# Weight splits of the first group moved to earlier steps, clock fillers taken out of the first three tiles

## The chip, the cores and the metric

One program on one core of a Trainium2 chip, launched once. The metric is device time in microseconds from start to end of the program. The engines are TensorE (PE), VectorE (DVE), ScalarE (ACT), GpSimd (POOL) and SyncE (SP), which only issues DMAs here. Each runs its own instructions in order and waits on semaphores for the others.

## The reference

Three layers, one behind the other, all float32:

```
# 1. attention with a decaying state, 4 batches, 8 heads, 768 positions, 48 wide
for t in range(S):
    cur = einsum('bhd,bhe->bhde', u[None] * kt, vt)
    y[:, :, t] = einsum('bhd,bhde->bhe', rt, state + cur)
    state = w[None, :, :, None] * state + einsum('bhd,bhe->bhde', kt, vt)
# 2. gated layer, 3072 tokens x 384, 1536 hidden
gate = 1 / (1 + exp(-(x @ w_gate)))
x = (gate * (x @ w_val)) @ w_out
# 3. eight experts, each token to the one with the largest logit
logits = normalized(x) @ normalized(expert_emb).T / tau
out[mask] = gate_w[mask] * (relu(x[mask] @ w1[e]) @ w2[e])
```

## The kernel before

**Tiles and groups.** The 3072 tokens are 24 tiles of 128 (6 per batch). Three tiles make a group; there are 8 groups, 0 to 7. The gated layer works on a group at a time, in 12 steps (`hidden_step`, f = 0 to 11, 128 hidden columns each), and then projects the three tiles (`project`, 12 chunks each). Between the steps of a group the attention of the next group's tiles is worked in: `att_of` gives step f the stage (f - 1) mod 4 of one of three tiles. Stage 0 scales k and r (`scale_k`, `scale_r` on VectorE; the k_tok product L575 and the two bonus products on GpSimd), stage 1 is the scores on TensorE (L1255, L1262) and the masks and the state on VectorE (L935 to L954), stage 2 is the output (L1278, L1286), the bonus (L588 on GpSimd) and the sum of both (L963, L969 on VectorE), stage 3 turns it (L1292) and splits it (L737 on ScalarE, L973 on VectorE). Group 0 has no earlier group: its tiles T=0, 1, 2 are worked alone before step 0 (the opening). Beside group 0's steps run tiles T=3, 4, 5.

**Split matmuls.** Every matmul of layer 2 is made of three, with each float32 operand split into a high part, as the matmul's fp32r type rounds it, and the remainder. A step has 18 of them (L1332): per three chunks of 128 rows, for gate and value, high x high, high x low and low x high. A step's chain is: TensorE, the sigmoid (L745, ScalarE), the product with the value (L1081, VectorE, called the gate below), the high part of the hidden row (L749, ScalarE) and its low part (L618, GpSimd). TensorE's step f waits for the gate of step f - 2, since they share PSUM banks; the sigmoid of step f waits for L618 of step f - 2.

**Weights of layer 2.** They come as pieces: g0 to g5 (w_gate), v0 to v5 (w_val), each 256 hidden columns wide and so first used by step f = 2j, o0 to o5 (w_out, two chunks of the projection each), and t0 to t5 (w_out turned, from which 12 small column products on TensorE, `logit_columns`, L1302, work out the router's weights). A piece is loaded by SP into a room ("s0", "h", "l3", ...; `PIECES` has the order and the room), which must be free of its former tenant. ScalarE copies its high part (`make_hi`, L796), then VectorE (g, v: `make_lo`, L1124) or GpSimd (o: L600) subtracts it for the low part; both together are called the split below. Three tables say at which step of group 0 the queue of each engine has which piece, behind the step's own work: `HI_AT` (ScalarE), `LO_AT` (VectorE), `LO_O_AT` (GpSimd). The step's own work on VectorE and GpSimd includes the attention stage; on GpSimd attention comes before L618, on VectorE it comes behind the gate. Step f = 2j on TensorE waits for the later of g_j's and v_j's VectorE splits (`lo_count`).

**The opening's order.** On VectorE, ahead of tile 0's stage 1, stand the squares of the expert embeddings, their scaling (L989 to L992) and the copy of the turned embeddings (L994). Then for each tile: scale_k of the next, the split of g0 or v0, stage 2, scale_r of the next, stage 3, stage 1 of the next. Stage 1 ends with the sum L957, which waits for GpSimd's bonus products. On TensorE: stage 1, two logit columns, stage 2, two more, stage 3 and four filler matmuls on the identity (`keep_clock`, L1375), which write a bank nobody reads.

## Time and profile before

| | us |
|---|---|
| three runs | 877.86, 878.61, 879.29 |
| median | 878.61 |
| the profiled execution | 877.35 |
| its span | 875.6 |
| mean granted TensorE clock | 0.975 |
| TensorE busy | 837.6 (96%) |
| VectorE busy | 440.1 (50%) |
| GpSimd busy | 423.1 (48%) |
| ScalarE busy | 297.2 (34%) |

The span is what the profile covers; the execution's own time has what lies around it, 1.75 us. In the chain of work that ended last TensorE has 88% of the span. The span in 40 slices of 21.9 us, in tenths busy:

```profile
PE   6778899999999999999999999998999999999995
DVE  6566545545545545545545543377367267265100
PEclk8688899999999999999999999999999999999998
DMA  9643212212212212212212210136344354354110
```

TensorE falls short of 9 tenths in the first five slices (0 to 109 us) and at the turn to the experts. The granted clock is under 9 tenths in the same first slices.

### The profile page before, as it was taken

To read this page: it belongs to the slowest core of one execution; us is meant where nothing else is said; L and a number is where in the kernel's file an instruction comes from. 1 tells how busy PE (TensorE), PEld (TensorE's weight loads), DVE (VectorE), ACT (ScalarE), POOL (GpSimd) and SP (SyncE) were. 2 spreads that over 40 slices of the span, in tenths; PEclk is the share of its full clock that TensorE was granted. 3 is DMA by queue.
4 is the path that set the end of the run, shared out by engine and by line. 5 is a ranking of instruction groups with operands and counts; after the bars stand their busy time and mean duration, and the time that the engine had idled before them with its cause. 6 is when DMAs were issued, how large, how long until landed. Compare 5 with 4: busy or idle time off the path is not lost.

```text
span 875.6 us, 20375 instructions
## 1 busy us (share of the span) xinstructions
PE 837.6 (96%) x7466; PEld 792.2 (90%) x7467; DVE 440.1 (50%) x1051; ACT 297.2 (34%) x610; POOL 423.1 (48%) x452
## 2 busy tenths in 40 slices
PE   6778899999999999999999999998999999999995
PEld 6777899999999999999999999987999989989995
DVE  6566545545545545545545543377367267265100
ACT  1143223223223223223223214333544444454442
POOL 3465516516516516516516513336566466466544
PEclk8688899999999999999999999999999999999998
DMA  9643212212212212212212210136344354354110
GB/s 279 218 149 112 74 48 82 69 48 79 71 48 76 75 48 75 75 49 74 76 48 75 69 47 19 38 117 197 109 144 142 109 156 143 98 157 141 50 36 30
DMA packets 78421, 82.04 MB, mean 94 GB/s; under 512 B 5816, under 2 KB 75648, under 8 KB 78352
## 3 DMA queue, kind: packets, MB, share of 16 engines
q1 hardware_dynamic: 65200, 60.29, 23.1%
q10 hardware_dynamic: 9216, 9.55, 3.8%
q0 software_dynamic: 3936, 11.23, 3.4%
q8 instruction: 49, 0.80, 0.4%
q14 instruction: 20, 0.16, 0.1%
HBM read 69.83 MB, written 12.01 MB: 93 GB/s over the span
## 4 chain that ended last, share of the span: by engine, by line
PE 88%; DVE 4%; issue 2%; ACTq 2%; POOL 2%; ACT 1%; DMA 1%; POOLq 0%; DVEq 0%
PE ps L1332 33%; PE ps L1353 16%; PE ps L1435 13%; PE ps L1420 13%; PE ps L1443 3%; PE ps L1255 2%; PE ps L1278 1%; DVE weights L1124 1%; PE ps L1262 1%; PE ps L1292 1%; PE ps L1400 1%; PE ps L1286 1%; PE ps L1375 1%; ACTq L370 1%; POOL weights L600 1%
## 5 line engine op out<-in xcount | busy, mean ns | idle before, releaser
L1332 PE MATMUL ps<-x_groups,weights 128*128 128x384 f32 x1728 | 321.9, 342 | 12.2 <-DVE weights L1124 12.2
L1332 PEld LDWEIGHTS ps<-x_groups,weights 128*128 128x128 f32 x1728 | 303.3, 191 | 14.9 <-issue 13.1
L618 POOL TENSOR_TENSOR hT<-gate,hT 128x384 fp32r<-128x384 f32 x96 | 104.1, 1087 | 144.4 <-ACT hT L749 144.4
L1353 PE MATMUL ps<-weights,hT 128*128 128x392 f32 x864 | 160.6, 344 | 0.0
L1353 PEld LDWEIGHTS ps<-weights,hT 128*128 128x128 f32 x864 | 152.6, 188 | 0.4
L1435 PE MATMUL ps<-weights,hT 128*128 x672 | 124.2, 339 | 1.7 <-ACT h_f L854 1.7
L1420 PE MATMUL ps<-weights,x_groups 128*128 (+1 forms) x504 | 122.8, 397 | 1.2 <-issue 1.2
L1081 DVE TENSOR_TENSOR gate<-ps,gate 128x384 f32<-128x384 f32 x96 | 53.5, 557 | 135.4 <-PE ps L1332 129.0
L1435 PEld LDWEIGHTS ps<-weights,hT 128*128 128x128 f32 x672 | 115.9, 188 | 2.0 <-issue 1.9
L1420 PEld LDWEIGHTS ps<-weights,x_groups 128*128 128x128 f32 x504 | 92.6, 188 | 20.5 <-issue 1.7
L1067 DVE CAST weights<-staged 128x768 fp32r<-128x768 f32 x56 | 49.3, 881 | 93.5 <-PE ps L1420 54.9
L749 ACT CAST hT<-gate 128x384 fp32r<-128x384 f32 x96 | 49.3, 514 | 124.1 <-DVE gate L1081 124.1
L1069 DVE TENSOR_TENSOR weights<-staged,weights 128x768 fp32r<-128x768 f32 x60 | 80.5, 1344 | 3.5 <-ACT weights L791 1.4
L623 POOL TENSOR_TENSOR top<-top,one_half 128x1 f32<-128x1 f32 x24 | 13.5, 563 | 134.9 <-ACT row L758 134.9
L745 ACT ACTIVATE gate<-ps 128x384 f32<-128x384 f32 x96 | 47.2, 491 | 90.5 <-PE ps L1332 77.4
L704 POOL TENSOR_TENSOR hT<-h_f,hT 128x512 fp32r<-128x512 f32 x56 | 72.2, 1308 | 2.7 <-ACT h_f L854 1.8
L758 ACT ACTIVATE row<-x 128x384 f32<-128x384 f32 x24 | 12.6, 527 | 117.3 <-DVE x L1001 117.3
L836 ACT ACTIVATE A_room<-ps 128x512 f32<-128x512 f32 x56 | 33.5, 599 | 46.4 <-PE ps L1420 45.5
L688 POOL COPY dest<-Z 128x1 int32 x28 | 9.4, 336 | 74.8 <-ACT k_in L859 74.8
L859 ACT COPY k_in<-ps 128x384 f32<-128x384 f32 x28 | 13.4, 478 | 92.0 <-PE ps L1435 92.0
L692 POOL DMA_INDIRECT out<-k_in,dest x28 | 29.9, 1066 | 23.7 <-POOL dest L688 22.2
L682 POOL TENSOR_TENSOR x_groups<-kT,x_groups 128x384 fp32r<-128x384 f32 x29 | 32.9, 1134 | 16.0 <-ACT kT L831 15.9
(183 smaller groups left out, 973.0 us busy)
## 6 DMA issues: line engine op xcount, KB each, us to landing
staged<-in_moe_w SPq DMA_DIRECT2D x60, 384.0 KB, 3.4
r_in<-routed ACTq DMA_DIRECT2D x30, 192.5 KB, 2.4
rk_raw<-in_rt SPq DMA_DIRECT2D x21, 256.0 KB, 3.6
rk_raw<-in_kt SPq DMA_DIRECT2D x21, 256.0 KB, 3.9
...
```

What stands on the lines that cost most here:

```text
L618: g.tensor_tensor(hT_lo[:, f, :], gate[:, f % 2, :], hT_hi[:, f, :].bitcast(F32), ALU.subtract).then_inc(hlo_ready, 1)
L704: g.tensor_tensor(eh_lo[:, c, :], h_f[:, c, :], eh_hi[:, c, :].bitcast(F32), ALU.subtract).then_inc(ehlo_ready, 1)
L745: s_.activation(gate[:, f % 2, :], ps[:, BG[f % 2], 0:GT], ACT.Sigmoid).then_inc(sig_ready, 1)
L749: s_.copy(hT_hi[:, f, :], gate[:, f % 2, :]).then_inc(hhi_ready, 1)
L836: s_.activation(h_rows[:, q * 512:(q + 1) * 512], ps[:, BH[q], :], ACT.Relu).then_inc(relu_ready, 1)
L1067: ve.tensor_copy(hi, raw).then_inc(ehi_step, 1)
L1069: ins = ve.tensor_tensor(lo, raw, hi.bitcast(F32), ALU.subtract)
L1081: ve.tensor_tensor(gate[:, f % 2, :], ps[:, BV[f % 2], 0:GT], gate[:, f % 2, :], ALU.mult).then_inc(h_ready, 1)
L1332: ins = te.matmul(ps[:, bank[f % 2], 0:GT], wt[:, c, fs], x[:, half, c, :], start=(c == 0 and m == 0), stop=(c == KC - 1 and m == 2))
L1353: ins = te.matmul(ps[:, BX2[i], 0:XW], h[:, f, ts], wt[:, f, :], start=(f == 0 and m == 0), stop=(f == FC - 1 and m == 2))
L1420: ins = te.matmul(ps[:, BH[q], :], x[:, c, :], columns(buf, o + c * EF + q * 512, 512), start=(c == 0 and m == 0), stop=(c == KC - 1 and m ...
L1435: ins = te.matmul(ps[:, BO, 0:DM], h[:, c, :], columns(buf, o + c * DM, DM), start=(ready is ehf_ready and c == 0 and m == 0), stop=(ready ...
```

## The change

Four things, no arithmetic among them:

1. The tables of group 0. The g and v splits stand at earlier steps than before on ScalarE and VectorE, the o splits at later steps than all but the last g and v ones. The o pieces now wait for the rooms s0, s1 and h instead of x0 to x2, and SP's order of loads follows.
2. The opening on VectorE. Stage 1 of tile 0 comes ahead of the scaling of the embeddings; the copy of the turned embeddings comes behind tile 0's stage 3; the splits of g0 and v0 stand ahead of the next tile's stage 1 instead of ahead of stage 2; the sum (`sum_bonus`) is taken out of stage 1 for these tiles, and for tiles 1 and 2 stands ahead of it. The embeddings lie in another buffer for that.
3. The opening on TensorE. The embeddings are turned behind tile 0's stage 3; the 12 logit columns come in tiles 1 and 2 (3, 2, then 3, 2, 2); the fillers of the three tiles are gone. The 16 + 8 fillers ahead of tile 0 stay.
4. ScalarE no longer waits for o2's split ahead of tile 3's stage 3, since no w_out piece lies in that room now.

```
-    HI_AT = {1: "g2 o0", 2: "o1 v2", 3: "o2 g3", 4: "v3", 5: "v4 o3", 6: "g4 o4", 7: "g5", 8: "v5 o5"}
-    LO_AT = {0: "g1 v1", 1: "g2", 3: "v2", 4: "g3 v3", 5: "v4", 7: "g4 g5", 8: "v5"}
-    LO_O_AT = {2: "o0 o1", 3: "o2", 6: "o3 o4", 8: "o5"}
+    HI_AT = {0: "g2 v2", 2: "g3", 3: "v3 v4", 4: "g4", 5: "o0 o1", 6: "g5 v5", 7: "o2 o3", 8: "o4", 9: "o5"}
+    LO_AT = {0: "g1 v1", 1: "g2 v2", 3: "g3", 4: "v3 v4", 5: "g4", 7: "g5 v5"}
+    LO_O_AT = {6: "o0 o1", 8: "o2 o3", 10: "o4", 11: "o5"}
...
-            load_pieces(PIECES[:17])
+            load_pieces(PIECES[:14])
             fetch(sp, 0, 3)
             fetch_v(sp, 0, 3)
-            load_pieces(PIECES[17:20])
+            load_pieces(PIECES[14:18])
             fetch(sp, 0, 4)
-            load_pieces(PIECES[20:21])
+            load_pieces(PIECES[18:19])
             fetch_v(sp, 0, 4)
-            load_pieces(PIECES[21:23])
+            load_pieces(PIECES[19:20])
             fetch(sp, 0, 5)
+            load_pieces(PIECES[20:23])
             fetch_v(sp, 0, 5)
             load_pieces(PIECES[23:])
...
                 if stage == 3:
-                    if isinstance(T, int) and T == TPG:
-                        act.wait_ge(*lo_count("o", 2))
                     act.wait_ge(y_turned, T + 1)
...
             hidden_step(0, 0)
+            for kind, j in pieces_at(HI_AT, 0):
+                make_hi(kind, j)
             batches(act, step)
...
-            attention(0, 0, 0, 1, 0)
             for i in range(TPG):
+                if i:
+                    make_lo("gv"[i - 1], 0)
+                    sum_bonus(i)
+                attention(0, i, i, 1, 0)
+                if i == 0:
+                    sum_bonus(0)
                 if i + 1 < TPG:
                     scale_k(0, i + 1)
-                    make_lo("gv"[i], 0)
+                if i == 0:
+                    scale_embeddings()
                 attention(0, i, i, 2, 0)
                 if i + 1 < TPG:
                     scale_r(0, i + 1)
                 attention(0, i, i, 3, 0)
-                if i + 1 < TPG:
-                    attention(0, i + 1, i + 1, 1, 0)
+                if i == 0:
+                    dve.wait_ge(en_t, 1)
+                    ve.tensor_copy(enT[:, :, :], ps[:, BX, 0:KC * E].rearrange("p (c e) -> p c e", c=KC)).then_inc(enT_ready, 1)
...
+            chunk = 0
             for i in range(TPG):
-                attention(0, i, i, 1)
-                if i == 0:
-                    turn_embeddings()
-                    pe.wait_ge(enT_ready, 1)
-                for c in range(4 * i, 4 * i + 2):
-                    logit_columns(c)
-                attention(0, i, i, 2)
-                for c in range(4 * i + 2, 4 * i + 4):
-                    logit_columns(c)
-                attention(0, i, i, 3)
-                keep_clock(BX2[1], 4)
+                for stage, chunks in ((1, 3), (2, 2), (3, 2)):
+                    attention(0, i, i, stage)
+                    if i == 0 and stage == 3:
+                        turn_embeddings()
+                        pe.wait_ge(enT_ready, 1)
+                    if i > 0 and (stage < 3 or i == TPG - 1):
+                        for c in range(chunk, chunk + chunks):
+                            logit_columns(c)
+                        chunk += chunks
             hidden_step(0, 0, 0, first=True)
```

In the changed kernel VectorE's lines stand 6 lower (L1124 is L1130), GpSimd's 1, TensorE's 13.

How the order moves, at two places. First GpSimd from step 6 of group 0 to the start of step 9. `hT` is the low part L618, `weights` a w_out split, `bonus` the bonus product of T=4, `k_tok` the k product of T=5. Before:

```order
L618 TENSOR_TENSOR hT<-gate,hT 128x384 x2
L600 TENSOR_TENSOR weights<-staged,weights 128x2x384 x2
L588 TENSOR_TENSOR bonus<-v_in,bonus_sum 128x384
L618 TENSOR_TENSOR hT<-gate,hT 128x384 x2
L600 TENSOR_TENSOR weights<-h_f,weights 128x2x384
L575 TENSOR_TENSOR k_tok<-k_in,pow_tok 128x8x48
```

Changed:

```order
L619 TENSOR_TENSOR hT<-gate,hT 128x384 x2
L601 TENSOR_TENSOR weights<-staged,weights 128x2x384 x2
L589 TENSOR_TENSOR bonus<-v_in,bonus_sum 128x384
L619 TENSOR_TENSOR hT<-gate,hT 128x384 x2
L601 TENSOR_TENSOR weights<-h_f,weights 128x2x384
L601 TENSOR_TENSOR weights<-staged,weights 128x2x384
L576 TENSOR_TENSOR k_tok<-k_in,pow_tok 128x8x48
```

The two splits ahead of the bonus are o0 and o1 instead of o3 and o4; ahead of k_tok there are two splits (o2, o3) instead of one (o5).

Second, VectorE in steps 1 to 3 of group 0. `gate` is the gate of a step, `weights` a g or v split, `kT` and `rT` T=3's scaled k and r, `A_room` the state and the masks, `bonus` the sums of T=3's output. Before:

```order
L918 TENSOR_TENSOR kT<-rk_raw,pow_k 128x512
L924 TENSOR_TENSOR rT<-rk_raw,pow_r 128x512
L1124 TENSOR_TENSOR weights<-first_room,weights 128x3x256
L1081 TENSOR_TENSOR gate<-ps,gate 128x384
L946 TENSOR_TENSOR A_room<-ps,Z 128x192
...
L963 TENSOR_TENSOR bonus<-ps,bonus 128x2x4x48
L969 TENSOR_TENSOR bonus<-ps,bonus 64x4x48 x2
L1124 TENSOR_TENSOR weights<-first_room,weights 128x3x256
L1081 TENSOR_TENSOR gate<-ps,gate 128x384
```

Changed:

```order
L924 TENSOR_TENSOR kT<-rk_raw,pow_k 128x512
L930 TENSOR_TENSOR rT<-rk_raw,pow_r 128x512
L1130 TENSOR_TENSOR weights<-first_room,weights 128x3x256 x2
L1087 TENSOR_TENSOR gate<-ps,gate 128x384
L952 TENSOR_TENSOR A_room<-ps,Z 128x192
...
L969 TENSOR_TENSOR bonus<-ps,bonus 128x2x4x48
L975 TENSOR_TENSOR bonus<-ps,bonus 64x4x48 x2
L1130 TENSOR_TENSOR weights<-staged,weights 128x3x256
L1087 TENSOR_TENSOR gate<-ps,gate 128x384
```

v2's split, which stood behind the bonus sums of step 3, now stands beside g2's in step 1, and g3's (from `staged`) has its place in step 3.

## Rows read from the trace of the kernel before

**Rows 1.** Windows, group 0 and group 1; busy us of PE, PEld, DVE, ACT, POOL, clock, DMA share, GB/s

```profile
43.76:128.85 85.09, 72.67 (x708) 69.52 (x708) 46.49 (x94) 26.95 (x51) 41.88 (x33) 0.90 0.32 98
128.85:194.79 65.94, 65.94 (x709) 63.52 (x708) 34.73 (x106) 18.96 (x41) 30.01 (x30) 1.00 0.22 66
```

**Rows 2.** Timeline of PE, steps 4, 6, 8: start, us, [idle before <-releaser]

```profile
66.89 5.46 PE L1332 MATMUL ps<-x_groups,weights 128*128 128x384 f32 x18 [5.80 <-DVE weights L1124]
...
77.39 3.39 PE L1332 MATMUL ps<-x_groups,weights 128*128 128x384 f32 x18 [1.58 <-DVE weights L1124]
...
90.83 4.50 PE L1332 MATMUL ps<-x_groups,weights 128*128 128x384 f32 x13 [4.57 <-DVE weights L1124]
```

**Rows 3.** Chain that ended last: start, us; steps 4 and 8 of group 0, one of group 1

```profile
66.89 5.46 PE ps L1332 x18
...
90.83 5.44 PE ps L1332 x18
...
139.48 3.33 PE ps L1332 x18
```

**Rows 4.** Timeline of POOL and DVE ahead of step 4

```profile
58.70 3.73 POOL L600 TENSOR_TENSOR weights<-group_room,weights 128x768 fp32r<-128x768 f32 x2
...
63.32 0.56 DVE L963 TENSOR_TENSOR bonus<-ps,bonus 128x384 f32<-128x384 f32 x1 [2.64 <-POOL bonus L588]
...
64.58 2.17 DVE L1124 TENSOR_TENSOR weights<-first_room,weights 128x768 fp32r<-128x768 f32 x1
```

**Rows 5.** Timeline of group 0: prices of splits, masks' last write, step 3, L618

```profile
54.85 1.76 DVE L1124 TENSOR_TENSOR weights<-first_room,weights 128x768 fp32r<-128x768 f32 x1
...
56.61 3.40 PE L1332 MATMUL ps<-x_groups,weights 128*128 128x384 f32 x18
...
57.71 1.02 POOL L618 TENSOR_TENSOR hT<-gate,hT 128x384 fp32r<-128x384 f32 x1 [0.22 <-ACT hT L749]
...
58.20 0.75 DVE L954 TENSOR_TENSOR Z<-Z,w_pow 128x192 f32<-128x192 f32 x1
...
78.58 1.50 DVE L924 TENSOR_TENSOR rT<-rk_raw,pow_r 128x512 f32<-128x512 f32 x1
...
89.72 0.96 DVE L1124 TENSOR_TENSOR weights<-h_f,weights 128x768 fp32r<-128x768 f32 x1
```

**Rows 6.** DMA issues, 40 to 110 us: KB each, median us to landing

```profile
staged<-in_moe_w_out SPq DMA_DIRECT2D x2, 384.0 KB, 3.9
```

**Rows 7.** DMA issues, 0 to 30 us: KB each, median us to landing

```profile
h_f<-in_moe_w_gate SPq DMA_DIRECT2D x1, 384.0 KB, 14.6
```

**Rows 8.** Windows, fillers of tile 0 and end of the first stall; columns as in rows 1

```profile
22.00:24.00 2.00, 1.23 (x6) 1.23 (x7) 1.59 (x4) 0.29 (x1) 1.32 (x3) 0.50 1.09 350
...
66.00:68.00 2.00, 1.11 (x4) 1.14 (x5) 0.74 (x1) 0.00 (x0) 0.00 (x0) 0.50 0.03 10
```

**Rows 9.** Timeline of the opening: scores of tile 0, embeddings, first read, logit columns

```profile
14.56 0.63 PE L1262 MATMUL ps<-v_in,k_tok 64*64 64x48 f32 x32
...
14.73 0.14 DVE L989 TENSOR_SCALAR tiny<-tiny 8x1 f32<-8x1 f32 x1 [0.75 <-POOL tiny L579]
...
17.48 0.35 DVE L944 COPY A_room<-ps 128x192 f32<-128x192 f32 x1
...
20.24 1.46 PE L1302 MATMUL ps<-enT,first_room 128*64 128x8 f32 x24
```

**Rows 10.** Chain that ended last, the opening: transposes of tiles 0, 1, 2, fillers

```profile
22.77 0.90 PE ps L1292 x3
23.68 1.71 PE ps L1375 x8
...
32.62 0.90 PE ps L1292 x3
...
41.50 0.90 PE ps L1292 x3
```

More of the change, by code:

```diff
@@ L67, in fused_kernel @@
               ("t", 4, "x1"), ("t", 5, "x2"), ("g", 1, "h"), ("v", 1, "l3"), ("g", 2, "l4"), ("v", 2, "l5"),
[2 rows of a table removed]
[2 rows of a table added]
     ROOM_OF = {(kind, j): room for kind, j, room in PIECES}
-    HI_SEQ = [("g", 0), ("v", 0), ("g", 1), ("v", 1), ("g", 2), ("o", 0), ("o", 1), ("v", 2), ("o", 2), ("g", 3),
-              ("v", 3), ("v", 4), ("o", 3), ("g", 4), ("o", 4), ("g", 5), ("v", 5), ("o", 5)]
+    HI_SEQ = [("g", 0), ("v", 0), ("g", 1), ("v", 1), ("g", 2), ("v", 2), ("g", 3), ("v", 3), ("v", 4), ("g", 4),
+              ("o", 0), ("o", 1), ("g", 5), ("v", 5), ("o", 2), ("o", 3), ("o", 4), ("o", 5)]
     LO_SEQ = [("g", 0), ("v", 0), ("g", 1), ("v", 1), ("g", 2), ("v", 2), ("g", 3), ("v", 3), ("v", 4), ("g", 4),
               ("g", 5), ("v", 5)]
-    HI_AT = {1: "g2 o0", 2: "o1 v2", 3: "o2 g3", 4: "v3", 5: "v4 o3", 6: "g4 o4", 7: "g5", 8: "v5 o5"}
-    LO_AT = {0: "g1 v1", 1: "g2", 3: "v2", 4: "g3 v3", 5: "v4", 7: "g4 g5", 8: "v5"}
-    LO_O_AT = {2: "o0 o1", 3: "o2", 6: "o3 o4", 8: "o5"}
+    HI_AT = {0: "g2 v2", 2: "g3", 3: "v3 v4", 4: "g4", 5: "o0 o1", 6: "g5 v5", 7: "o2 o3", 8: "o4", 9: "o5"}
+    LO_AT = {0: "g1 v1", 1: "g2 v2", 3: "g3", 4: "v3 v4", 5: "g4", 7: "g5 v5"}
+    LO_O_AT = {6: "o0 o1", 8: "o2 o3", 10: "o4", 11: "o5"}
     PRE, SPLIT = len(HI_SEQ), len(LO_SEQ)
-    RING = 6
+    RING = 8
     assert PRE == NWO + 2 * NWG and SPLIT == 2 * NWG and EPC % 2 == 0
@@ L154, in fused_kernel @@
         y = bonus[:, :, :].rearrange("p h d -> p (h d)")
-        enc = A_room[0:E, 0:DM]
         bonus_sum = sb("bonus_sum", [P, H])
@@ L165, in fused_kernel @@
         row = sb("row", [P, 2, ROW])
+        enc = row[0:E, 1, 0:DM]
         prio = sb("prio", [P, E])
@@ L913, in _, with sum_bonus @@
             w128 = w_pow[:, 7, :]
+            def sum_bonus(T):
+                dve.wait_ge(rk_step, T * 2 + 2)
+                ve.tensor_reduce(bonus_sum[:, :], bonus[:, :, :], AX_X, ALU.add).then_inc(sum_ready, 1)
             def scale_k(b, c):
@@ L955, in attention @@
                                          ALU.mult).then_inc(z_ready, 1)
-                    dve.wait_ge(rk_step, T * 2 + 2)
-                    ve.tensor_reduce(bonus_sum[:, :], bonus[:, :, :], AX_X, ALU.add).then_inc(sum_ready, 1)
+                    if not isinstance(T, int) or T >= TPG:
+                        sum_bonus(T)
                 elif stage == 2:
@@ L987, in _, with scale_embeddings @@
             ve.tensor_reduce(tiny[0:E, 1:2], x2[0:E, 0:DM], AX_X, ALU.add).then_inc(en_squares, 1)
-            dve.wait_ge(en_norm, 1)
-            link(ve.tensor_scalar(tiny[0:E, 2:3], tiny[0:E, 5:6], 1e-6, None, ALU.add))
-            link(ve.tensor_tensor(tiny[0:E, 3:4], tiny[0:E, 2:3], tiny[0:E, 0:1], ALU.mult))
-            link(ve.reciprocal(tiny[0:E, 4:5], tiny[0:E, 3:4]))
-            ve.tensor_scalar(enc[:, :], enc[:, :], tiny[0:E, 4:5], None, ALU.mult).then_inc(en_ready, 1)
-            dve.wait_ge(en_t, 1)
-            ve.tensor_copy(enT[:, :, :], ps[:, BX, 0:KC * E].rearrange("p (c e) -> p c e", c=KC)).then_inc(enT_ready, 1)
+            def scale_embeddings():
+                dve.wait_ge(en_norm, 1)
+                link(ve.tensor_scalar(tiny[0:E, 2:3], tiny[0:E, 5:6], 1e-6, None, ALU.add))
+                link(ve.tensor_tensor(tiny[0:E, 3:4], tiny[0:E, 2:3], tiny[0:E, 0:1], ALU.mult))
+                link(ve.reciprocal(tiny[0:E, 4:5], tiny[0:E, 3:4]))
+                ve.tensor_scalar(enc[:, :], enc[:, :], tiny[0:E, 4:5], None, ALU.mult).then_inc(en_ready, 1)
             def choose(G, i):
@@ L1380, in _ @@
             keep_clock(BC, 8)
+            chunk = 0
             for i in range(TPG):
-                attention(0, i, i, 1)
-                if i == 0:
-                    turn_embeddings()
-                    pe.wait_ge(enT_ready, 1)
-                for c in range(4 * i, 4 * i + 2):
-                    logit_columns(c)
-                attention(0, i, i, 2)
-                for c in range(4 * i + 2, 4 * i + 4):
-                    logit_columns(c)
-                attention(0, i, i, 3)
-                keep_clock(BX2[1], 4)
+                for stage, chunks in ((1, 3), (2, 2), (3, 2)):
[7 more added lines that the diff above has]
+                        chunk += chunks
+            assert chunk == FC
             hidden_step(0, 0, 0, first=True)
```

4 rows, old and new, of the table PIECES are left out of this document.

## The prediction

> **What bounds the kernel now.** Two stretches lie before the point from which TensorE never waits: the opening (0 to 43.76 us, three attention tiles, one after the other) and group 0 (43.76 to 128.85). I read first the windows by group: group 0 takes 85.09 us, group 1, with the same matmuls, 65.94 us, with TensorE busy all of it at a granted clock of 1.00 [rows 1]. So at most 19.2 us can be won in group 0, and nothing behind it, since later groups are already full.
>
> Second, TensorE's timeline in group 0: it idles 5.80 us ahead of step 4, 1.58 ahead of step 6 and 4.57 ahead of step 8, always for a VectorE split (L1124) [rows 2], 11.95 us together. Third, the chain: the two long stalls leave the clock down, so step 4 takes 5.46 us and step 8 5.44, where a step costs 3.33 [rows 3]; the granted clock there is 0.50, that is 1.2 GHz, after the idle time of 60 to 66 us [rows 8]. That is 2.13 + 2.11 = 4.24 us more. A 1.58 us gap costs no clock: step 6 takes 3.39 [rows 2].
>
> Why step 4 starts late is seen on GpSimd and VectorE: two output splits (3.73 us) stand ahead of the bonus product L588, VectorE's L963 waits for it (2.64 us), and v2's split, queued behind L963, ends only at 66.75, when step 4 starts [rows 4]. The stall ahead of step 8 is the same with o3, o4 and g4.
>
> **Group 0, what goes.** In the changed order g2 and v2 are split in step 1, g3 in step 3, v3 and v4 in step 4, g4 in step 5, g5 and v5 in step 7, so none of the three steps finds its split behind a bonus wait of the same step. GpSimd has no output split before step 6. All three stalls and both slow steps go: 11.95 + 4.24 = **16.2 us**.
>
> **Group 0, what comes.** The splits still cost VectorE the same; 1.76 us each where GpSimd works beside them, 0.96 where it rests [rows 5]. They now stand ahead of other things:
> - Step 1: v2's split is added behind g2's. T=3's masks, whose last write ends at 58.95 now, end 1.76 later, at 60.7; TensorE is there at 60.01 [rows 5]. Wait 0.7 to 1.2, I take 0.9. GpSimd has lost its 3.73 us there, so the bonus of T=3 is then in time.
> - Step 4 to 5: gate, L973, two splits (3.5), gate, scale_k, scale_r (1.0 + 1.5, the second [rows 5]). From step 4's start: 3.3 + 0.6 + 0.8 + 3.5 + 0.6 + 2.5 = 11.3, against steps 4 to 6 and a turn of 0.3 on TensorE, 10.3 to 10.4. Wait 0.9 for T=4's scores. Step 6's own split ends at about 6.5, ahead of 7.0.
> - Steps 6 to 8: o0 and o1 stand ahead of T=4's bonus as o3 and o4 do now. From step 6: scale_r ends at 4.3, g4's split and the gate at 6.6, copy and L618 1.6 (L618 1.02 [rows 5]), splits 3.7, bonus 0.8, L963 and L969 1.25: 14.0 to 14.2, against TensorE at step 8's end 13.1. Its transposes wait 1.0, no longer its hidden steps.
> - Steps 8 to 9: a new place. Now one output split (o5) lies between L618 of step 8 and T=5's k_tok product, then two (o2, o3). From step 6's start as above: g5 and v5 0.96 each after 14.2, gate, copy, L618: 18.2; splits 3.7 to 4.8; k_tok 1.0: 22.9 to 24. TensorE wants k_tok at 21.7 (13.1, the wait of 1.0, the turn 0.3, steps 9 and 10, 0.6 of score matmuls). Wait 1.9 (1.2 to 3).
> - Small ones, steps 2 and 11: 0.3. The last output split ends about 1 us ahead of its use in the projection: nothing, or 1 if late.
>
> Sum of new waits 0.9 + 0.9 + 1.0 + 1.9 + 0.3 = **5.0 us** (3 to 8), none near the length that took the clock down. Group 0 gains 16.2 − 5.0 = 11.2.
>
> The w_out loads now form a chain, each waiting for a consumed room. A load of this kind lands in 3.9 us [rows 6]; at that the copies of o3 and o5 hold ScalarE for a few us, which delays sigmoids of steps 8 and 10 but no step two behind them. SP's other moves (T=3's loads up to 10 us earlier, since the three w_out loads ahead of them are gone; T=4's loads behind v5) stay inside slack.
>
> The split price needs a rule weighed. The row says 1.76 beside a GpSimd instruction and 0.96 alone [rows 5], a slowing of both, not a block. The Trainium skill (SBUF — State Buffer, Who interferes with whom) says that a VectorE instruction with two SBUF inputs and a GpSimd instruction that reads SBUF hold a shared port as an exclusive lock, so the later one fully blocks. By that a split behind a 1.0 us product would take about 1.96, the waits of steps 1 and 4 would grow by some 0.2 and 0.4, and the sum would be 0.6 us less gain.
>
> **The opening.** Tile 0: scores are there at 15.19, but VectorE, in the embedding work from 14.73 on, starts tile 0's first read at 17.48 [rows 9]. Now that read comes first: 2.29 earlier. The four embedding operations (2.2 us from 14.73 to 16.94) then stand ahead of L963 instead, and the 1.1 us split and enT's copy leave it: 15.2 + 1.9 (reads, masks, sum) + 0.6 (kT) + 2.2 = 19.9, plus 1.25 gives the transposes at 21.2, where they stand at 22.77 [rows 10]: 1.6 earlier (0.8 to 2.5).
>
> Tile to tile: now 9.85 and 8.88 us between transposes, 1.71 of each in fillers on the chain [rows 10]. Changed, VectorE sets it: L973 done 2.0 after the transposes start, split 1.0 to 1.6, sum 0.5, four mask and state operations 1.55: 5.1 to 5.7; TensorE's second stage 1.1; L963, L969 1.25: 8.1 for the second turn. In the first, TensorE also waits for enT's copy (at 2.2), and 36 logit matmuls at a rate of 24 in 1.46 us [rows 9] follow its scores (4.15 + 2.2 = 6.35), so second stage from 6.3: 8.7 to 9.6. I take 9.2 and 8.3: 0.65 and 0.6 earlier. The last fillers ahead of step 0: L973 is the limit anyhow, 0.3. Opening: 1.6 + 0.65 + 0.6 + 0.3 = **3.1 us** (1 to 5).
>
> **Sum.** 11.2 + 3.1 = 14.3 us. The profiled execution took 877.35 (span 875.6), so 863.05 for it; the median of the three runs is 878.61, 1.26 above, so **864.3**.
>
> **Rivals.**
> - *The clock.* The fillers ran at 0.50 with TensorE 1.23 of 2 us busy [rows 8]; they may still be what brings it to full speed for each tile's second stage. Without them the second stage costs about 1.0 more in each tile, and one of the new waits may grow past 3 us and take the clock down once (2.1 + 1.5). For it: four waits share GpSimd and VectorE. Against: no single one is worked out above 3. Gain 8 to 11, time 869. In a sentence of its own: the Trainium skill (TensorE: Matmul & The Clock Gate, What's actually happening) has the default state as throttled and activity as what releases it, by which removing fillers speaks against this change. Chance 0.17.
> - *The clock stays up from the last tile into step 0*, as logit matmuls fill what was idle, and port contention is milder: steps 0 and 1 save 1.8, the waits 1 to 2. Gain 17.5, time 861. Chance 0.10.
> - *The chain of w_out loads decides (slower).* ScalarE's queue is in order: behind the copy of o3 (step 7) and of o5 (step 9) stand the sigmoids that TensorE's banks wait for. In the opening a load of the same size took 14.6 us to land [rows 7]. At that, two places lose 14.6 − 3.9 = 10.7 each, less 2 of slack: +19.4 − 14.3 = +5, time 884. It turns slower from a landing of 3.9 + (14.3 + 2) / 2 = 12 us. Against it: by step 6 the loads are few, and landed in 3.9 [rows 6]. Chance 0.03.
> - *It moves nothing,* because another wait of equal length already stands behind each (the bonus product, TensorE's own transposes): the time stays at 878.6. Against: each wait named by the profile is for a split. Chance 0.02.
>
> **How the numbers follow.** Forecast 0.68, rivals as above. The likeliest gives 864.3; its own bounds (new waits 3 to 8, opening 1 to 5) give 860.5 to 869, which also takes in most of the two clock cases. 0.2% is 1.8 us, about what a measurement of this kernel can tell from no change. Faster 0.95, same 0.02, slower 0.03.
>
> **What would show it.** In the changed profile TensorE's idle time for splits in group 0 is under 1 us instead of 12; step 0 starts at about 40.7; group 0 lasts about 74; no 18-matmul step behind step 0 takes over 4 us; new idle times of 1 to 2 us appear ahead of L1255/L1262, L1278 and the transposes, the longest for T=5's k_tok. A stall of over 3 us with a 0.50 clock behind it, or ScalarE waiting long for a w_out load, would make the prediction wrong; so would an opening that is no shorter.

## The result and the profile after

| | before | changed |
|---|---|---|
| median of the runs made side by side, us | 878.95 (877.86 to 879.74, 4 runs) | 869.56 (869.07 to 871.41, 4 runs) |
| profiled execution, us | 877.35 | 869.66 |
| its span, us, mean granted clock | 875.6, 0.975 | 867.6, 0.977 |

The ratio is 0.9898, 95% interval 0.9879 to 0.9916: 9 us faster, where 14.3 were forecast. The median lies 0.56 us above the upper end of the stated range (860.5 to 869; the bounds given for its parts add up to 869.4), and within 0.6 us of the 869 of the rival "the clock".

The page of the changed kernel, its row for the hidden steps (columns: busy us, mean ns | idle time ahead, its releaser). Before, idle time for VectorE splits was 12 us [rows 2]:

```profile
L1345 PE MATMUL ps<-x_groups,weights 128*128 128x384 f32 x1728 | 320.2, 341 | 0.2 <-DVE weights L1130 0.2
```

Windows of group 0 and group 1 in the changed kernel, columns as in [rows 1]:

```profile
42.24:118.81 76.57, 71.80 (x710) 68.48 (x709) 47.04 (x94) 27.18 (x52) 41.64 (x33) 0.93 0.37 110
118.81:184.80 65.99, 65.99 (x709) 63.56 (x708) 34.77 (x107) 18.96 (x41) 30.02 (x30) 1.00 0.22 66
```

Group 0 went from 85.09 to 76.57 us (8.5 won, 11.2 forecast), and group 1 is as it was. It starts 10 us earlier than before, of which the profiled execution keeps 8 at its end. The rest, from group 1's start on, which no edit here touches, took 746.9 us in the profile of before, 748.8 in this one and 747.1 to 749.4 in those of the experiments: a profile of one execution is good to some 2 us there, and the profile of before has the lowest of all.

The timeline of TensorE in group 0 of the changed kernel: the waits that are left.

```profile
42.35 8.27 PE L1345 MATMUL ps<-x_groups,weights 128*128 128x384 f32 x36
50.88 3.39 PE L1345 MATMUL ps<-x_groups,weights 128*128 128x384 f32 x18 [0.25 <-DVE weights L1130]
...
59.34 0.26 PE L1291 MATMUL ps<-v_in,A_room 64*64 64x48 f32 x2 [0.67 <-issue]
...
71.58 0.69 PE L1268 MATMUL ps<-rT,kT 64*64 64x64 f32 x32 [1.08 <-DVE rT L930]
...
81.24 0.55 PE L1305 MATMUL ps<-ident,bonus 128*128 128x128 f32 x3 [0.76 <-DVE bonus L975]
...
89.92 0.69 PE L1268 MATMUL ps<-rT,kT 64*64 64x64 f32 x32 [1.86 <-DVE rT L930]
90.78 1.09 PE L1275 MATMUL ps<-v_in,k_tok 64*64 64x48 f32 x16 [0.16 <-POOL k_tok L576]
91.80 5.93 PE L1345 MATMUL ps<-x_groups,weights 128*128 128x384 f32 x18
```

None of the three long stalls of [rows 2] is left. In their place stand 0.25 + 0.67 + 1.08 + 0.76 + 1.86 + 0.16 = 4.8 us of short waits (the 0.25 ahead of step 2 is not new: 0.24 stood there before). For the 0.67 the profile names no releaser; VectorE's last write of T=3's masks ends at 59.24 us, just ahead of 59.34. But the last row, step 11, takes 5.93 us and not 3.4. The windows around it say why (the clock is the last number but two):

```profile
88.00:90.00 2.00, 0.14 (x5) 0.08 (x8) 1.86 (x1) 0.00 (x0) 2.00 (x2) 1.00 0.85 222
90.00:92.00 2.00, 1.84 (x49) 1.61 (x50) 0.27 (x1) 1.22 (x2) 1.92 (x3) 0.63 0.83 237
92.00:94.00 2.00, 2.00 (x7) 2.00 (x8) 1.67 (x5) 0.52 (x1) 2.00 (x3) 0.50 0.60 191
```

Behind the wait of 1.86 us the granted clock goes from 1.00 (2.4 GHz) to 0.50 (1.2 GHz), and step 11 runs at half speed for most of its time. What TensorE waited for there is on VectorE and GpSimd (timelines of both):

```profile
85.81 1.84 DVE L924 TENSOR_TENSOR kT<-rk_raw,pow_k 128x512 f32<-128x512 f32 x1
87.57 2.29 DVE L930 TENSOR_TENSOR rT<-rk_raw,pow_r 128x512 f32<-128x512 f32 x1
```

```profile
85.23 1.87 POOL L601 TENSOR_TENSOR weights<-h_f,weights 128x768 fp32r<-128x768 f32 x1
87.06 2.26 POOL L601 TENSOR_TENSOR weights<-staged,weights 128x768 fp32r<-128x768 f32 x1
89.28 1.45 POOL L576 TENSOR_TENSOR k_tok<-k_in,pow_tok 128x384 f32<-128x384 f32 x1
```

scale_k (L924) ends at 87.65, 0.55 us behind the first GpSimd split (87.10); scale_r (L930) ends at 89.86, 0.54 behind the second (89.32). In the opening, at 30.63 us with GpSimd at rest, the same L930 takes 0.69. So the two output splits o2 and o3 made scale_r late. They made k_tok (L576) late too: it stands behind both and ends at 90.73. The 0.16 that the timeline shows for it is only what was left of that wait. Steps 9 and 10 end at 88.06 us. Had scale_r been in time, the scores could have started then and the k_tok matmuls about 0.5 later, and TensorE would have waited 1.3 to 2.1 us for k_tok instead of 1.86 + 0.16 (an estimate from these rows; the 1.3 is with L601 and L576 as short as alone, 1.85 and 1.02 us).

The opening. Timeline of TensorE in the changed kernel, from tile 0's transposes on:

```profile
20.25 0.90 PE L1305 MATMUL ps<-ident,bonus 128*128 128x128 f32 x3 [2.46 <-DVE bonus L975]
23.44 1.13 PE L1268 MATMUL ps<-rT,kT 64*64 64x64 f32 x32 [1.88 <-DVE enT L1149]
25.32 2.09 PE L1315 MATMUL ps<-enT,first_room 128*64 128x8 f32 x36
27.35 1.11 PE L1291 MATMUL ps<-first_room,A_room 64*64 64x48 f32 x32
...
29.24 0.91 PE L1315 MATMUL ps<-enT,first_room 128*64 128x8 f32 x13
...
30.93 0.90 PE L1305 MATMUL ps<-ident,bonus 128*128 128x128 f32 x3
...
36.80 1.15 PE L1291 MATMUL ps<-first_room,A_room 64*64 64x48 f32 x32 [1.06 <-DVE A_room L941]
...
38.73 1.45 PE L1315 MATMUL ps<-enT,group_room 128*64 128x8 f32 x24
40.14 0.90 PE L1305 MATMUL ps<-ident,bonus 128*128 128x128 f32 x3
```

Against [rows 10], with tiles 1 and 2 from the changed kernel's chain: tile 0's transposes 22.77 → 20.25, tile 1's 32.62 → 31.0, tile 2's 41.50 → 40.2, step 0 43.76 → 42.35. What tile 0 won, 2.5 us, shrinks to 1.4. The chain says what tile 1's scores waited for:

```profile
19.38 1.28 ACT L802
...
20.87 1.46 ACT weights L795 x2
22.33 0.39 ACT x_groups L736
...
22.74 0.56 DVE x_groups L979
23.30 0.10 DVE enT L1149
```

VectorE's copy of enT stands behind L979, which waits for ScalarE's L736, which stands behind two high-part copies (L795) and a table load (L802). And the granted clock is 0.50 from 16 to 46 us. That shows in the second stages of tiles 1 and 2, from the first L1291 to the logit matmuls behind: 27.35 to 29.24 and 36.80 to 38.73, 1.9 us each. In the profile of before the same stage of tile 1 took 1.08 us:

```profile
28.97 0.68 PE L1278 MATMUL ps<-first_room,A_room 64*64 64x48 f32 x32 [0.93 <-DVE A_room L935]
...
30.05 1.12 PE L1302 MATMUL ps<-enT,group_room 128*64 128x8 f32 x24
```

The granted clock from 28 to 30 us is 1.00 in the profile of before and 0.50 in the changed kernel's.

ScalarE's waits between 60 and 110 us, for the rival about the w_out loads (us in total, times, longest):

```profile
ACT weights L795 <- DMA h_f<-in_moe_w_out: 4.0, 1, 4.0
ACT weights L795 <- DMA staged<-in_moe_w_out: 3.0, 1, 3.0
```

The loads do hold ScalarE, as worked out, but no hidden step waits for a sigmoid: no such wait stands in TensorE's timeline.

### The profile page after: what moved, and what is told of

Same layout as the page of the kernel before. It is cut to its first block, busy times and chain, and to the rows that moved or that the text cites. A ratio compares the mean times of both kernels' runs of the same rounds, so it can differ in the third digit from the quotient of the medians.

```text
span 867.6 us, 20325 instructions
## 1 busy us (share of the span) xinstructions
PE 835.4 (96%) x7442; PEld 789.1 (91%) x7443; DVE 440.1 (51%) x1051; ACT 297.4 (34%) x610; POOL 423.6 (49%) x452
## 4 chain that ended last, share of the span: by engine, by line
PE 86%; DVE 4%; POOL 3%; issue 2%; ACTq 2%; ACT 1%; DMA 1%; POOLq 0%; DVEq 0%; SPq 0%
PE ps L1345 32%; PE ps L1366 17%; PE ps L1448 14%; PE ps L1433 13%; PE ps L1456 3%; PE ps L1291 2%; PE ps L1268 1%; PE ps L1299 1%; PE ps L1275 1%; PE ps L1413 1%; ACTq L370 1%; PE ps L1305 1%; POOL weights L601 1%; PE ps L1315 1%; DVE weights L1130 1%
## 5 line engine op out<-in xcount | busy, mean ns | idle before, releaser
L1087 DVE TENSOR_TENSOR gate<-ps,gate 128x384 f32<-128x384 f32 x96 | 53.5, 557 | 129.2 <-PE ps L1345 119.6
L1075 DVE TENSOR_TENSOR weights<-staged,weights 128x768 fp32r<-128x768 f32 x60 | 83.0, 1386 | 3.5 <-ACT weights L790 1.4
L744 ACT ACTIVATE gate<-ps 128x384 f32<-128x384 f32 x96 | 47.2, 491 | 76.6 <-PE ps L1345 63.3
```

Source lines behind the costliest of these rows:

```text
L744: s_.activation(gate[:, f % 2, :], ps[:, BG[f % 2], 0:GT], ACT.Sigmoid).then_inc(sig_ready, 1)
L1075: ins = ve.tensor_tensor(lo, raw, hi.bitcast(F32), ALU.subtract)
L1087: ve.tensor_tensor(gate[:, f % 2, :], ps[:, BV[f % 2], 0:GT], gate[:, f % 2, :], ALU.mult).then_inc(h_ready, 1)
```

## The experiments

Times are medians; ratios are to the kernel before, run beside each experiment on the same chip, with the 95% interval. The kernel before had medians from 876.57 to 878.95 us there, so that experiments made at different times are compared by their ratios. 0.001 is 0.9 us. Diffs are against the changed kernel.

**The two halves alone.** `tables_only` keeps the opening of before (fillers, order of VectorE) with the changed split tables; `opening_only` is the reverse (the rooms, SP's order and ScalarE's wait go with the tables):

```diff
-    HI_AT = {0: "g2 v2", 2: "g3", 3: "v3 v4", 4: "g4", 5: "o0 o1", 6: "g5 v5", 7: "o2 o3", 8: "o4", 9: "o5"}
-    LO_AT = {0: "g1 v1", 1: "g2 v2", 3: "g3", 4: "v3 v4", 5: "g4", 7: "g5 v5"}
-    LO_O_AT = {6: "o0 o1", 8: "o2 o3", 10: "o4", 11: "o5"}
+    HI_AT = {1: "g2 o0", 2: "o1 v2", 3: "o2 g3", 4: "v3", 5: "v4 o3", 6: "g4 o4", 7: "g5", 8: "v5 o5"}
+    LO_AT = {0: "g1 v1", 1: "g2", 3: "v2", 4: "g3 v3", 5: "v4", 7: "g4 g5", 8: "v5"}
+    LO_O_AT = {2: "o0 o1", 3: "o2", 6: "o3 o4", 8: "o5"}
```

> The opening of the kernel before, with the tables of group 0, the rooms and SP's order of the change. Theory A (the two parts add): in the profile of the change group 0 lasts 76.6 us instead of 85.1, so this kernel gains 8.5 of the 9.4 us, time about 870.4, and step 0 starts at 43.8 as before. Rival B (the parts depend on each other: T=3's inputs and the clock that the opening leaves behind matter for group 0): group 0 differs from 76.6 us by more than 1 us, and the time lies outside 869.4 to 871.4.

> The opening of the change, with the tables of group 0 of the kernel before. Theory A (they add): step 0 starts at 42.4 instead of 43.8, group 0 lasts 85.1, gain 1.4, time about 877.5. Rival B: the opening alone brings 3 us or nothing, time under 876 or over 878.5.

Measured: tables_only 869.12 us, 0.9908 (0.9889 to 0.9926). opening_only 877.43 us, 1.0004 (0.9994 to 1.0015), though its step 0 starts at 42.51, 1.25 us earlier than in the profile of before. Alone, the opening's part is worth at most 0.5 us by its interval. Its 877.43 is the 877.5 of theory A only because the kernel before ran at 876.57 beside it: no gain of 1.4 is there. The tables alone give 8.1 us by their ratio where theory A had 8.5, but their profile is not the one that it described: step 0 starts at 42.72 (43.8 expected) and group 0 lasts 73.2 us instead of 76.6, as rival B had it, because the clock is up into step 0 (steps 0 and 1 take 6.48 us, not 8.27) and step 11 takes 4.95 us and not 5.93.

**The fillers again.** One line in the loop over the first tiles:

```diff
+                keep_clock(BX2[1], 4)
```

> The change with the four filler matmuls behind each of the first three tiles put back (nothing reads what they write). Theory A (the clock): the opening of the change gained only 1.4 of the 3.1 us forecast because TensorE stays at a granted clock of 0.50 from 16 to 46 us; with the fillers the clock is at 1.00 in the second stage of tiles 1 and 2 and the 36 logit matmuls take 1.3 us instead of 2.0, which pays back about what the fillers cost: time within 1 us of the change. Rival B (VectorE's and GpSimd's order sets the turns and the clock costs little): each filler block adds 1 to 1.7 us at tiles 0 and 1 and nothing at tile 2, time 2 to 3.5 us over the change.

Measured: 868.65 us, 0.9909 (0.9894 to 0.9923). The clock is up in tile 2 (0.96 at 38 to 40 us) and 24 logit matmuls take 0.85 us instead of 1.45, but step 0 starts only at 45.91. Step 11 took 3.40 in its profile. So the opening of this profile is 3.6 us longer than the changed kernel's, about as rival B had it, and the time is within 1 us, as theory A had it: the step 11 of 3.40 us instead of 5.93 gives 2.5 back. The fillers do not pay for themselves in the opening.

**enT's copy earlier.** On VectorE the copy is put ahead of tile 0's stage 3:

```diff
+                attention(0, i, i, 3, 0)
...
-                attention(0, i, i, 3, 0)
```

> The change with VectorE's copy of the turned embeddings put ahead of tile 0's stage 3 instead of behind it. In the change TensorE waited 1.88 us for that copy, since it stood behind a split that waited for ScalarE, whose queue was held by DMA issues, a table load and two weight copies until 22.3 us. Theory A (the opening's lost gain is this queue order): tile 1's scores start at 21.7 instead of 23.4 us, the next transposes 0.8 to 1.5 us earlier, step 0 at about 41.3. Rival B (the opening is bound by TensorE at a granted clock of 0.50, or by VectorE's split and sum): the scores start earlier, step 0 by less than 0.4 us.

Measured: 868.01 us, 0.9887 (0.987 to 0.9905). That is 1 us better than the changed kernel's ratio, with intervals that overlap. Timeline of TensorE: the scores of tile 1 wait 0.28 and start 0.8 us earlier, and what stands behind them 0.7 (step 0 at 41.65).

```profile
21.03 0.90 PE L1305 MATMUL ps<-ident,bonus 128*128 128x128 f32 x3 [4.08 <-DVE bonus L975]
22.62 1.13 PE L1268 MATMUL ps<-rT,kT 64*64 64x64 f32 x32 [0.28 <-DVE enT L1148]
...
30.25 0.90 PE L1305 MATMUL ps<-ident,bonus 128*128 128x128 f32 x3
```

The turn from tile 0 to tile 1 reads 9.22 us here, the 9.2 of the forecast, but by luck: the transposes of tile 0 stand 0.8 later. In the eight profiles with the changed kernel's own opening they start anywhere from 20.25 to 21.23 us, and tile 1's scores at 23.2 to 23.6 in all eight, since the copy sets them.

**Fillers only where TensorE idles**, in the gaps of tile 0:

```diff
+                    if i == 0 and stage < 3:
+                        keep_clock(BX2[1], 4 if stage == 1 else 6)
```

> The change with 4 + 6 filler matmuls (nothing reads what they write) put where TensorE idles in tile 0, behind its stages 1 and 2, and none on the chain. Theory A (the clock, let down at 16 us by that idle time, costs the opening 1.5 to 2.5 us): the granted clock is 1.00 in tile 1's stage 2, its logit matmuls take 1.3 us instead of 2.0 and stage 2 1.1 instead of 1.9, step 0 starts 1.5 to 2.5 us earlier. Rival B (the clock falls at tile 1 all the same, or the order on VectorE and GpSimd sets the turns): step 0 within 0.7 us of the change's 42.4.

Measured: 869.09 us, 0.9899 (0.9885 to 0.9914). Its windows show the clock high until tile 0's end and down in the wait for enT (2.43 us here). Step 0 starts at 43.46, 1.1 us later than in the changed kernel and not earlier: tile 1's second stage holds a pause of 0.99 us, for which the profile names no releaser. Neither theory had that.

```profile
20.00:22.00 2.00, 0.82 (x6) 0.57 (x6) 1.22 (x2) 1.99 (x4) 1.89 (x2) 0.91 1.11 329
22.00:24.00 2.00, 0.57 (x20) 0.57 (x24) 1.27 (x3) 0.70 (x2) 1.10 (x2) 0.50 1.08 360
```

**The logit columns spread 2, 2, 2** over the stages of tiles 1 and 2, with enT's copy early:

```diff
-                for stage, chunks in ((1, 3), (2, 2), (3, 2)):
+                for stage, chunks in ((1, 2), (2, 2), (3, 2)):
...
-                    if i > 0 and (stage < 3 or i == TPG - 1):
+                    if i > 0:
```

> The change with the early copy, and the 12 logit columns as 2, 2, 2 in tile 1 and 2, 2, 2 in tile 2 instead of 3, 2, 0 and 3, 2, 2. Theory A (at 1.2 GHz the three columns behind the scores, 2.1 us, and the two behind stage 2, 1.5 to 1.8 us, lie on TensorE's chain in tile 1): stage 2 of each tile starts up to 0.7 us earlier, and the two behind tile 1's transposes push its follower by as much as they take off or less: step 0 within 0.7 us either way of 41.5 to 41.65. Rival B (VectorE's chain has the slack): step 0 0.7 to 1.5 us earlier.

Measured: 867.77 us, 0.9878 (0.9858 to 0.9897), as enT_early; step 0 at 41.90, as theory A had it. Where TensorE had no logit matmuls to do in stage 1, it waited for VectorE instead (0.94 and 0.33 us).

**o3's split two steps later**, so that one GpSimd split, not two, stands beside scale_k and scale_r of T=5:

```diff
-    LO_O_AT = {6: "o0 o1", 8: "o2 o3", 10: "o4", 11: "o5"}
+    LO_O_AT = {6: "o0 o1", 8: "o2", 10: "o3 o4", 11: "o5"}
```

> The change with o3's split moved on GpSimd from step 8 to step 10. Theory A (T=5's wait is GpSimd's and VectorE's load from two splits in a row): k_tok comes about 2 us earlier, scale_r is slowed for a shorter time, TensorE's wait ahead of T=5's scores falls from 2.7 to under 1 us, the clock stays at 1.00 and step 11 takes 3.3 instead of 5.9 us: 3.5 to 4.5 us off the change, time 865 to 866. Rival B (the wait is VectorE's scale_r alone, which stands behind a gate that waits for ScalarE, itself held by the copy of o5): the wait stays over 1.5 us and the clock falls as well, gain under 1 us.

Measured: 865.68 us, 0.987 (0.9854 to 0.9885). By the ratios that is 2.5 us better than the changed kernel; theory A had 3.5 to 4.5, and its 865 to 866 is met because the kernel before was faster beside this run. The wait is 1.05 and step 11 takes 3.40; the projection then waits 0.94 for o5. Timeline of TensorE:

```profile
89.92 0.69 PE L1268 MATMUL ps<-rT,kT 64*64 64x64 f32 x32 [1.05 <-DVE rT L930]
91.00 3.40 PE L1345 MATMUL ps<-x_groups,weights 128*128 128x384 f32 x18
```

**Six fillers ahead of T=5's scores**, which leave every wait of VectorE and GpSimd as it is and only keep TensorE at work:

```diff
+                    if G == 0 and f == 10:
+                        keep_clock(BX, 6)
```

> The change with six filler matmuls ahead of T=5's scores in step 10 of group 0, where TensorE idles 1.86 us; nobody reads what they write. Theory A (that idle time, with the small score matmuls behind it, lets the clock down, and step 11 then takes 5.9 us instead of 3.4 in most executions): step 11 takes 3.4, group 0 is 1.5 to 2.5 us shorter, ratio 0.987 to 0.988 where the change has 0.9898. Rival B (the clock falls seldom, and the profile of the change caught it by chance): ratio 0.9895 to 0.990.

Measured: 867.36 us, 0.9877 (0.9859 to 0.9896). Idle 0.53 us, clock 1.00, step 11 as fast as the others (timeline of TensorE):

```profile
90.20 0.69 PE L1268 MATMUL ps<-rT,kT 64*64 64x64 f32 x32 [0.53 <-DVE rT L930]
91.07 0.67 PE L1275 MATMUL ps<-v_in,k_tok 64*64 64x48 f32 x16 [0.17 <-POOL k_tok L576]
91.67 3.40 PE L1345 MATMUL ps<-x_groups,weights 128*128 128x384 f32 x18
```

The scores start 8.69 us behind step 8's transposes (8.68 in the changed kernel), so no releaser came earlier. Group 0 is 2.5 us shorter than in the changed kernel, as much as step 11 gives. The ratio is 1.1 to 1.8 us better than the two of the changed kernel, as theory A had it, with intervals that overlap; and one profile alone can't show the cause, since four profiles with the wait left as it was also have a fast step 11 (below).

**The output splits into GpSimd's idle slots**, alone and with the g and v splits spread too:

```diff
+    LO_O_AT = {5: "o0", 6: "o1", 7: "o2", 8: "o3", 10: "o4", 11: "o5"}
```

```diff
+    LO_AT = {0: "g1 v1", 1: "g2 v2", 3: "g3", 4: "v3", 5: "v4", 6: "g4", 7: "g5 v5"}
```

> The change with GpSimd's splits of the output weight spread over its idle times: o0 in step 5, o1 in 6, o2 in 7, o3 in 8, o4 in 10, o5 in 11, instead of two in step 6 and two in step 8. Theory A (GpSimd's pairs of splits make the waits of T=4's bonus, 0.76 us, and of T=5's scores, 2.0 us plus the clock behind it): the first goes, the second falls to about 1.0 as when o3 is moved to step 10, and no wait for o5 takes its place: 3.5 to 5 us off the change, ratio to the kernel before 0.984 to 0.987. Rival B (moved work only moves the wait, as for o5 with o3 in step 10): no better than that kernel's 0.987.

> As the run before, and VectorE's splits of v4 and g4 each a step later (v3 in step 4, v4 in 5, g4 in 6). Theory A (T=4's scores wait 1.08 us for scale_r, which stands behind two splits): that wait goes and step 8 does not yet wait for g4, 1 us off the run before. Rival B (VectorE's work is only shifted): step 8 waits for g4 by 0.5 to 1.5 us and the time stays or grows.

Measured: o_in_idle 866.85 us, 0.9877 (0.9861 to 0.9894); o_idle_v_split 867.65, 0.9879 (0.9861 to 0.9897). In o_in_idle the wait ahead of step 8's transposes goes; in o_idle_v_split that ahead of T=4's scores falls to 0.36, and step 10 waits 0.92 us for a gate instead. The wait of T=5 stays in both, at 2.01 and 2.00, and the times are those of rival B. The idle slots were not free: in o_in_idle VectorE's pair g5, v5 takes 3.11 us where it takes 1.82 beside a resting GpSimd. And in o_in_idle the wait of 2.01 did not bring the clock down, in o_idle_v_split 2.00 did (step 11 5.62 us).

**The best parts together**: o3_later with enT_early (o3_enT), and the same with the gap fillers (o3_enT_gaps).

> Both changes that helped alone: o3's split in step 10 (ratio 0.987 to the kernel before) and the early copy of the turned embeddings (0.9887), where the change has 0.9898. Theory A (one acts in group 0, the other in the opening, so they add): ratio 0.9859, step 0 at about 41.5. Rival B (the clock's history ties them): ratio 0.987 or more.

> The run before with the 4 + 6 fillers in tile 0's idle times. With fillers alone the clock was at 1.00 until 21.5 us and fell at once, since TensorE waited 2.43 us for the copy. Theory A (the clock costs the opening 1.5 to 2.5 us once nothing else holds TensorE): the clock is now at 1.00 through tile 1, step 0 starts 1 to 2.5 us ahead of the run before, ratio 0.983 to 0.985. Rival B (64-wide attention matmuls with VectorE's work between them don't hold the clock, whatever stands ahead of them): the clock falls in tile 1, step 0 and ratio as in the run before.

Measured: 865.81 us, 0.9862 (0.9845 to 0.9878), as theory A had it (0.9859), and 865.03 us, 0.9852 (0.9835 to 0.987). The second beats the changed kernel by 3.3 to 4.0 us by the ratios. The two differ by 0.9 us, within their intervals, and step 0 starts at 41.88 and 41.60, so that rival B of the second stands: the clock is at 1.00 until 22 us and at 0.50 from 22 to 24.

**Once more, side by side**: the change, its tables alone, o_in_idle, and the last version with o2 in step 7.

```diff
-    LO_O_AT = {6: "o0 o1", 8: "o2", 10: "o3 o4", 11: "o5"}
+    LO_O_AT = {6: "o0 o1", 7: "o2", 10: "o3 o4", 11: "o5"}
```

> The change as it stands, once more, to see whether the fall of the clock behind T=5's wait comes back in another execution, and for a time beside tables_again. Theory A (the opening's part of the change is worth nothing measurable): within 1.5 us of tables_again, ratio 0.989 to 0.992. Theory B (it is worth the 1.4 us that the first profile showed, and something hid it): 1.5 to 3 us under tables_again. On the clock: if the fall depends on the program alone, step 11 takes 5.5 to 6.0 us again; if it is a matter of chance in each execution, 3.4 us is as likely.

> The change's tables with the old opening, once more, beside the change. Theory A: 868 to 870 us, within 1.5 us of change_again. Theory B: 1.5 to 3 us above it. On the clock: step 11 took 4.95 us in its first profile behind a wait of 1.85; fixed by the program: 4.5 to 5.3 again; chance: anything from 3.4 to 5.9.

> The output splits in GpSimd's idle slots, once more. Its first profile had a wait of 2.01 us ahead of T=5's scores, longer than the change's 1.86, and yet step 11 took 3.42 at a clock of 1.00. If what decides is fixed by the program (what TensorE did around the gap, and not the gap's length alone), step 11 takes 3.4 again and the time is 866 to 867.5; if it is chance, the profile may show 5 to 6 us, and the single times should lie apart in two heaps some 2 us from each other.

> The best version so far (o3 two steps later, enT's copy earlier, fillers in the gaps of tile 0) with o2's split in step 7 instead of step 8. Theory A (T=5's wait is the sum of what GpSimd and VectorE do to each other between steps 8 and 10): the wait of 1.05 ahead of T=5's scores falls to under 0.4, and the wait of 0.73 ahead of T=4's transposes stays or grows by up to 0.8, since o2 may stand ahead of T=4's bonus; 864.5 to 865.5. Theory B (scale_r is late by VectorE's own queue): both waits as they were, 865.

| | median, us | ratio (95%) | wait ahead of T=5's scores, step 11 |
|---|---|---|---|
| change_again | 868.41 | 0.989 (0.9871 to 0.9909) | 1.85, 5.77 |
| tables_again | 868.10 | 0.9909 (0.9886 to 0.9933) | 1.85, 3.40 (4.95 in tables_only) |
| o_in_idle_again | 867.02 | 0.9882 (0.9864 to 0.9899) | 1.98, 3.40 |
| o2_step7 | 864.04 | 0.9843 (0.9827 to 0.9859) | 1.16, 3.41 |

The medians of the change and of its tables alone are 0.3 us apart. By the ratios the change is 1.7 us better here and 0.9 in the first pair, with intervals that overlap (two of the six executions of tables_again took 872.1 and 873.0 us). So what the opening's part brings on top of the tables is not resolved: between nothing and some 2 us. The same program, tables_only and tables_again, had its clock up at 40 to 42 us in one execution and down in the other:

```profile
40.00:42.00 2.00, 1.29 (x19) 1.21 (x16) 0.88 (x3) 0.45 (x2) 0.00 (x0) 1.00 0.00 0
```

```profile
40.00:42.00 2.00, 2.00 (x68) 1.91 (x68) 0.35 (x2) 0.00 (x0) 0.83 (x1) 0.50 0.00 0
```

Its step 0 started at 42.72 and at 45.53, and its step 11 took 4.95 and 3.40 us. The two other programs that were run twice repeated their step 11 (5.93 and 5.77 in the change, 3.42 and 3.40 in o_in_idle), so that the program alone does not decide it, at least for the one. Without the fillers it starts at 42.35 (changed), 42.51 (opening_only) and 42.52 (change_again), with the clock at 0.50 each time.

o2_step7 has the lowest time, 0.8 us under o3_enT_gaps by the ratios and within the intervals. The wait ahead of T=5's scores did not fall to under 0.4 as theory A had it. Timelines of VectorE and GpSimd:

```profile
87.69 0.98 DVE L924 TENSOR_TENSOR kT<-rk_raw,pow_k 128x512 f32<-128x512 f32 x1
88.60 1.49 DVE L930 TENSOR_TENSOR rT<-rk_raw,pow_r 128x512 f32<-128x512 f32 x1
```

```profile
87.11 1.02 POOL L576 TENSOR_TENSOR k_tok<-k_in,pow_tok 128x384 f32<-128x384 f32 x1
88.08 1.45 POOL L583 TENSOR_TENSOR bonus<-k_in,r_in 128x384 f32<-128x384 f32 x1
```

Other GpSimd work (k_tok and the bonus product) has taken the place of the splits, and scale_k and scale_r again end 0.54 and 0.56 us behind it. And the pair begins later, 5.85 us behind the start of step 8's transposes instead of 4.58 (o3_later): o2's split now stands beside g5's and v5's, which take 3.10 us instead of 1.83. That is 1.3 us lost, where scale_k had won 0.85 (1.83 to 0.98).

## Why the forecast was partly right

**Group 0, what goes (16.2): right.** All three stalls and both slow steps of [rows 2, 3] are gone; the page has 0.2 us of idle time for splits left.

**Group 0, what comes (5.0): right, 4.8, one cause incomplete.** T=3's masks 0.67 (forecast 0.9), T=4's scores 1.08 (0.9), step 8's transposes 0.76 (1.0), T=5 1.86 + 0.16 (1.9), small ones 0.25 (0.3). For T=5 I had named k_tok; the profile names scale_r. By the rows both were late by the same two splits (k_tok ends at 90.73, 0.87 behind scale_r), and o3_later, with one of them moved, has 0.8 us less wait for scale_r and none for k_tok. That the sum came out as forecast is in part luck: it was worked out with GpSimd's splits alone, and scale_k and scale_r at their usual length.

**The step that failed: "none near the length that took the clock down".** I took the 1.58 us gap of [rows 2], behind which a step ran at 3.39, as proof that gaps of 1 to 2 us are free. The wait of 1.86 us was followed by step 11 at 5.9 us instead of 3.4: 2.5 us lost. In filler_T5, with the gap filled, the step is fast again. But the fall does not follow each time: of 16 profiles with the new tables, counting the changed kernel's, the five with a wait of 0.5 to 1.2 us kept the clock; of eleven with 1.85 to 2.01, seven lost it (step 11 at 4.6 to 5.9) and four did not. The same program did both (tables_only, tables_again). If the length of the wait played no part, all five short ones would be among the nine that kept it with a chance of 0.03 only; so the wait is the cause as far as these runs can show. What decides among the eleven is open. With the 2.5 us group 0 comes to 16.2 − 4.8 − 2.5 = 8.9, measured 8.5; the small rest is the matmuls of T=5 ahead of step 11, partly at half clock (L1275, 1.09 us, where filler_T5 has 0.67).

**The opening (3.1): wrong; the step that failed is "TensorE's second stage 1.1".** Forecast and measured starts: tile 0's transposes 21.2 and 20.25, tile 1's 30.4 and 31.0, tile 2's 38.7 and 40.2, step 0 40.7 and 42.35. Tile 0 came earlier than forecast, but nothing follows from it, since tile 1's scores wait for enT's copy. That came at 23.4 us, just where the forecast put it (21.2 + 2.2); in part luck, because its chain runs over ScalarE and not behind the transposes. Up to the second stage of tile 1 the forecast holds (27.5, measured 27.35). Then both second stages take 1.9 us at a clock of 0.50 instead of 1.1, which is the price at 1.00: 0.8 + 0.8 of the 1.7 us that step 0 is late. In fillers_back the stage of tile 2, with the clock up, takes 1.08 again. So this was the first half of the rival "the clock", and the forecast had priced the stage as if the clock stayed. TensorE's wait of 1.06 in the second turn, with GpSimd's L585 at 1.67 us beside VectorE's split, is no extra: the stage starts 5.8 us behind the transposes, 5.1 to 5.7 forecast.

Of the 1.2 to 1.4 us by which step 0 starts earlier in the profiles, opening_only shows at most 0.5 in the times. Two reasons are in the traces. The opening with fillers is not one length but 42.7 to 45.5 us, by where the clock stands, so that one profile of before was a weak base for a term of 3 us. And an early step 0 at a low clock is a slow one: steps 0 and 1 take 7.8 to 9.3 us in the eight profiles with the changed kernel's opening, and 6.5 to 8.2 in the three with the old one. At the start of step 2 the old opening has 49.45, 52.24 and 52.67 us, the new one 50.73 to 52.14, with means of 51.5 and 51.3: nothing is left of the lead, though three profiles are a thin base.

**Rivals.** "The clock" gave the time, 869, and both its halves happened: one new wait that takes the clock down (at 1.86 us and not past 3), and slower second stages (1.9 us each instead of 1.1; the fillers that cured one of them cost more in the opening than they brought). It had too small a chance beside a forecast that excluded it by one row. "The clock stays up into step 0" did not happen: steps 0 and 1 take 8.27 us, as before (8.24); it did in tables_only, with the fillers. The w_out loads landed in 3.3 us (3.9 in [rows 6], 12 needed).

**The split price.** I took 1.76 beside GpSimd as "a slowing of both, not a block". That reading was wrong, though its size hardly mattered. In before the same rows show it, set beside GpSimd's:

```profile
54.46 1.34 POOL L584 TENSOR_TENSOR bonus<-bonus,u_tok 128x384 f32<-128x384 f32 x1
...
64.13 1.80 POOL L600 TENSOR_TENSOR weights<-group_room,weights 128x768 fp32r<-128x768 f32 x1
```

The split that begins at 54.85 ends at 56.61 [rows 5], 0.81 us behind the GpSimd product (55.80); v2's ends at 66.75 [rows 4], 0.82 behind GpSimd's split (65.93). In the changed kernel the four 768-wide splits with a row of their own that begin while GpSimd works end 0.80 to 0.82 us behind it, and the 512-wide scale_k and scale_r of group 0, all six, 0.54 to 0.56. A fixed rest behind the other's end, whatever the length, is a block. This is what the Trainium skill says (SBUF — State Buffer, Who interferes with whom): the port pair that VectorE shares with GpSimd is an exclusive lock, and a VectorE instruction with two SBUF inputs contends for it with a GpSimd instruction that reads SBUF. The trace agrees: 0.54 to 0.56 and 0.80 to 0.82 us, as above. The gate products L1087, which read PSUM, take 0.54 to 0.56 us beside GpSimd as alone, and two of them end 0.30 and 0.43 us ahead of the GpSimd product beside them.
